# Another hand-written order for the head of a fused attention and gated-MoE kernel, and its last three token tiles grouped one by one

## The chip, the cores and the metric

One core of a Trainium2 chip (trn2). The metric is the time of one execution on the device in microseconds. Three runs of the kernel before took 551.12, 551.37 and 553.83 us; their median, 551.37 us, is the time before. All data are float32; the big products are made of float32r parts.

## What is computed

The reference, cut to what matters:

```python
# q, k, v: (4, 8, 576, 64)
out_d = softmax(scale * mean4(q) @ mean4(k).T) @ mean4(v)        # sequence pooled by 4
out_local = softmax(where(|i - j| < 4, scale * q @ k.T, -1e9)) @ v
x = tokens(repeat4(out_d) + out_local)                           # (2304, 512)
x = (sigmoid(x @ w_gate) * (x @ w_val)) @ w_out                  # d_ff = 1536
logits = x @ phi                                                 # 8 experts x 4 slots
slot_in = softmax(logits, axis=tokens).T @ x
slot_out[e] = relu(slot_in[e] @ w1[e]) @ w2[e]                   # w1, w2: 8 x 512 x 1024
out = softmax(logits, axis=slots) @ slot_out                     # (2304, 512)
```

## The kernel before, in words

**Attention.** The 4 x 8 heads are handled as 16 pairs of heads. A pair is a chain of steps: `Q0 Q1 K0 K1` transpose q and k to head-major form (TensorE, L937; copied out by ScalarE), `pool_Q pool_K pool_V` add up groups of four on GpSimd (L639 to L651), `S0 S1` are the local scores (L944), `Sd` the pooled ones (L952), `mx0 mx1 mxd` the mask and the maxima on VectorE, `ex exd` the exponents on ScalarE, `norm norm_d` the sums and quotients on VectorE, `PT PdT` transposes of the probabilities (L962 to L979), and `PVd PV0 PV1` the products with v (L973, L989), whose sum VectorE writes into `xraw`, a ring of 1152 tokens.

**Feed-forward.** Tokens come in 18 tiles of 128. `xs:i` splits a tile of x into a high and a low part (`xhl`). `gate:i.c` and `val:i.c` are 12 matmuls of 512 columns each (L1036), for one of three 512-wide chunks c of the 1536 columns: x-high by w-high, x-high by w-low, x-low by w-high. ScalarE takes the tanh of gate (L730), VectorE multiplies with val into `hid` (L851). `TR:i.c` transposes hid back (L1046) into `hT`. The weights w_gate and w_val come in 12 pieces of 512 KB (`w_in`), of which `w_hi` (ScalarE, L658) and `w_lo` (VectorE, L839) make the two parts.

**Routing.** w_out is never applied to the tokens. In the head, w_out's 12 pieces (`wo_in`) are transposed (`WT`, L995) and multiplied by phi (`GP`, L1002), and `GS` (L1010) brings that into `gmat`, so that `LG` (L1060) gives a group's logits from `hT` directly. For a group of one or two tiles `LS` (L1070) spreads the logits, VectorE takes a running maximum (L859 to L863), ScalarE the exponents and the factor `alpha` (L752 to L658), `ELT` (L1076) transposes the exponents back, and `SL` (L1085) adds up weighted `hid` per slot, which VectorE adds to `acc` (L879). `LG0` is a part of a group's logits done ahead. The groups before: seven pairs of tiles, then tile 14, tile 15, and tiles 16 and 17 together.

**Experts.** 32 tiles of 1 MB of w1 and w2 stream into 24 places (`ew_low`, `ew_high`), 21 at first and 11 again into places already used. The places lie over the memory of the earlier phases: `wait_place` (L573) lets SP issue a tile once that memory is dead, `first_places` gives the sequence of places. In numbers of places, 7 to 18 are the split weights of gate and val, chunk by chunk, 19 and 20 are `xhl`, and 21 to 23 hT, hid and small tiles. After the last group come the transposes of `acc` (L1110), the product with w_out (L1117), then for each expert `up` (L1136), a transpose (L1146) and the second product (L1154), and in the end 18 output tiles (L1178).

**What sets the order.** Every engine walks one list of steps and takes its part of each. The list begins with the texts `HEAD` (pairs 0 to 4, all of w_out, most weight pieces) and `FIRST_TILE` (token tile 0), both written out step by step. `program_steps` (L72) makes the rest: an alternation of gate and val with the attention of the later pairs between, `put` places the routing steps by hand, and the last three tiles have an order of their own. Loads of the head are steps too: SP issues them in list order, and each waits on SP for what it overwrites (`q_in` for `Q1`, `k_in` for `K1`, `v_in` for `PV1` of the pair before, `v4_in` for `pool_V`, `wo_in` for `WT` four pieces back). `place` (L177) deals PSUM banks to the steps in list order, seven in the head, four after it. `keep_clock` (L901) issues dummy matmuls on TensorE.

```python
put(place_of[("val", (i, c))] + 1, ("TR", (i, c)))
...
def load_wo_piece(sp, f):
    if f >= WO_STAGES:
        wait_unit(sp, ("WT", f - WO_STAGES))
...
for s in head + body[:k]:
    load_step(sp, s)
```

## Time and profile before

| | us |
|---|---|
| median of three runs (551.12, 551.37, 553.83) | 551.37 |
| the profiled execution, its own time | 553.79 |
| its span, from first to last instruction | 552.0 |
| TensorE busy | 528.6 |
| VectorE busy | 225.4 |
| ScalarE busy | 195.8 |
| GpSimd busy | 106.8 |
| mean granted TensorE clock, share of full speed | 0.985 |

The span has three stretches: the head with the first token tile (to 83 us), the feed-forward with attention between (to 484 us), and the routing's end, the experts and the output (to 552 us). An engine's busy time counts all its instructions, with pipelined matmuls counted once. A long wait of an engine that is not the one the end hangs on costs nothing. The profiled execution is longer by 1.8 us than its span, and every duration read from it belongs to its own 553.79 us.

### The profile page before, as it was taken

Reading aid. Unit: us, or ns where it says so; the run is one execution under the profiler, and the core shown is the slowest. Engines: PE = TensorE matmul, PEld = TensorE weight load, DVE = VectorE, ACT = ScalarE, POOL = GpSimd, SP = SyncE. Lnnn points to the kernel's source line nnn. Section 1 sums busy time; section 2 is a strip of 40 time slices with the busy share of each in tenths; the row PEclk is TensorE's granted clock in tenths of the full one; section 3 lists DMA queues with packets and bytes.
Section 4 is the critical chain, followed back from the end, with each engine's and each line's share of the span. In section 5 each row is a group of like instructions: output and inputs, shape, how many; then the busy total and the mean of one; then the engine's idle time right before and its main releaser. Section 6 shows DMA issues by size and latency. Waiting matters only on the chain.

```text
span 552.0 us, 11786 instructions
## 1 busy us (share of the span) xinstructions
PE 528.6 (96%) x4770; PEld 404.1 (73%) x4770; DVE 225.4 (41%) x484; ACT 195.8 (35%) x530; POOL 106.8 (19%) x171
## 2 busy tenths in 40 slices
PE   5989999999999999999999999999999999999982
PEld 4768778877887787878777877878777788854431
DVE  0977965343643446253353527432223110140113
ACT  3757754242443243424233425233122212231022
POOL 8556253221212123112121212100000000000000
PEclk9979999999999999999999999999999999999997
DMA  9966963210311122011111110107006077599959
GB/s 207 231 159 153 341 131 89 67 44 14 77 47 45 45 45 67 23 47 44 47 44 45 45 47 0 27 1 287 18 0 213 17 262 275 215 397 394 400 192 342
DMA packets 86709, 71.00 MB, mean 129 GB/s; under 512 B 61312, under 2 KB 65920, under 8 KB 86656
## 3 DMA queue, kind: packets, MB, share of 16 engines
q1 hardware_dynamic: 86656, 70.25, 41.5%
q8 instruction: 38, 0.62, 0.5%
q14 instruction: 15, 0.12, 0.1%
HBM read 65.52 MB, written 4.72 MB: 127 GB/s over the span
## 4 chain that ended last, share of the span: by engine, by line
PE 85%; DMA 6%; SPq 2%; DVE 2%; issue 1%; ACT 1%; POOL 1%; DVEq 0%; ACTq 0%; POOLq 0%
PE gateb L1036 26%; PE valb L1036 26%; PE unitb L1046 4%; DMA ew_low<-in_moe_w_dram 3%; PE unitb L944 3%; PE unitb L989 3%; PE unitb L937 3%; PE unitb L1060 2%; PE unitb L1085 2%; DMA v<-in_v_dram 2%; PE unitb L973 2%; PE unitb L952 1%; PE unitb L1136 1%; PE unitb L979 1%; PE gateb L1154 1%
## 5 line engine op out<-in xcount | busy, mean ns | idle before, releaser
L1036 PE MATMUL valb<-w_hl,xhl 128*128 128x512 f32 x648 | 162.1, 399 | 0.0
L1036 PE MATMUL gateb<-w_hl,xhl 128*128 128x512 f32 x648 | 161.7, 398 | 0.0
L1036 PEld LDWEIGHTS gateb<-w_hl,xhl 128*128 128x128 f32 x648 | 118.3, 188 | 28.9 <-issue 4.1
L1036 PEld LDWEIGHTS valb<-w_hl,xhl 128*128 128x128 f32 x648 | 118.4, 188 | 25.0 <-issue 1.4
L851 DVE SCALAR_TENSOR_TENSOR hid<-hid,valb 128x512 f32<-128x512 f32 x54 | 37.1, 687 | 121.8 <-PE valb L1036 121.7
L730 ACT ACTIVATE hid<-gateb 128x512 f32<-128x512 f32 x54 | 32.2, 597 | 143.6 <-PE gateb L1036 143.6
L647 POOL TENSOR_TENSOR vd<-v 72x256 f32<-72x256 f32 x16 | 13.6, 850 | 103.6 <-PE unitb L973 87.5
L843 DVE TENSOR_TENSOR xhl<-xraw,xhl 128x512 fp32r<-128x512 f32 x18 | 12.8, 709 | 48.9 <-ACT xhl L658 48.8
L1046 PE MATMUL unitb<-ident,hid 128*128 128x128 f32 x216 | 31.9, 272 | 0.0
L658 ACT ACTIVATE hT<-unitb 128x512 f32<-128x512 f32 x54 | 31.7, 592 | 0.3 <-PE unitb L1046 0.3
L1046 PEld LDWEIGHTS unitb<-ident,hid 128*128 128x128 f32 x216 | 26.5, 140 | 6.8 <-issue 0.4
L639 POOL TENSOR_TENSOR qd<-qT 128x144 f32<-128x144 f32 x16 | 9.5, 596 | 98.1 <-ACT qT L658 97.9
L682 ACT ACTIVATE probd<-unitb,negd 128x144 f32<-128x144 f32 x33 | 12.2, 377 | 34.2 <-DVE negd L793 34.2
L642 POOL TENSOR_TENSOR qd<-qd,qT 128x144 f32<-128x144 f32 x32 | 22.7, 710 | 2.5
L780 DVE TENSOR_TENSOR prob<-unitb,mask 128x350 f32<-128x350 f32 (+1 forms) x24 | 11.5, 481 | 25.0 <-PE unitb L944 24.7
L658 ACT ACTIVATE probT<-unitb 70x64 f32<-70x64 f32 (+1 forms) x45 | 15.1, 338 | 16.4 <-PE unitb L979 16.4
L642 POOL TENSOR_TENSOR kd<-kd,kT 128x144 f32<-128x144 f32 x32 | 19.4, 607 | 2.5
L989 PE MATMUL unitb<-probT,vloc 70*64 70x64 f32 x528 | 18.3, 222 | 0.0
L989 PEld LDWEIGHTS unitb<-probT,vloc 70*64 70x64 f32 x528 | 17.6, 138 | 0.5 <-issue 0.4
L834 DVE TENSOR_TENSOR xraw<-unitb,outd 128x384 f32<-128x384 f32 (+1 forms) x29 | 12.2, 455 | 12.8 <-PE unitb L989 12.8
L944 PEld LDWEIGHTS unitb<-kT,qT 64*64 64x64 f32 x432 | 15.0, 138 | 3.3 <-issue 3.2
L944 PE MATMUL unitb<-kT,qT 64*64 64x70 f32 x432 | 16.9, 229 | 0.0
(179 smaller groups left out, 659.3 us busy)
## 6 DMA issues: line engine op xcount, KB each, us to landing
ew_low<-in_moe_w_dram SPq DMA_DIRECT2D x19, 1024.0 KB, 12.1
ew_high<-in_moe_w_dram SPq DMA_DIRECT2D x13, 1024.0 KB, 8.2
qtok<-in_q_dram SPq DMA_DIRECT2D x32, 144.0 KB, 2.7
ktok<-in_k_dram SPq DMA_DIRECT2D x32, 144.0 KB, 2.9
v<-in_v_dram SPq DMA_DIRECT2D x32, 144.0 KB
out_dram<-outs SPq DMA_DIRECT2D x18, 256.0 KB, 3.0
vloc<-in_v_dram SPq DMA_DIRECT2D x32, 112.0 KB
xraw<-in_moe_w_out_dram SPq DMA_DIRECT2D x12, 256.0 KB, 4.7
```

What stands on the lines that cost most here:

```text
L642: nc.gpsimd.tensor_tensor(dst, dst, src[j], ALU.add).then_inc(step if j == 2 else done, 1)
L647: nc.gpsimd.tensor_tensor(vd[:, :, :, :], v4[:, :, :, 0, :], v4[:, :, :, 1, :], ALU.add).then_inc(vd_step, 1)
L658: return nc.scalar.activation(dst, src, ACT.Copy, scale=scale)
L682: last = nc.scalar.activation(probd[:, t, :], ub[:, t * SD:(t + 1) * SD], ACT.Exp, bias=negd[:, t:t + 1], accum_out=smd[:, t:t + 1])
L730: nc.scalar.activation(hid[:, i % NH, c * CW:(c + 1) * CW], gateb[n % 2][:, :], ACT.Tanh, scale=0.5)\
L843: nc.vector.tensor_tensor(xhl[:, arg % NX, 1, :, :], xraw[:, :, tok:tok + P], xhl[:, arg % NX, 0, :, :].bitcast(F32), ALU.subtract).then_i ...
L851: nc.vector.scalar_tensor_tensor(out=here, in0=here, scalar=1.0, in1=valb[n % 2][:, :], op0=ALU.add, op1=ALU.mult).then_inc(hid_done, 1)
L937: last = nc.tensor.transpose(ub[:, (t - t0) * TT:(t - t0 + 1) * TT], tok[:, t, :, :].rearrange("p h d -> p (h d)"), ident[0:TT, 0:TT])
L944: last = mm(ub[rows, (t - t0) * KW:(t - t0 + 1) * KW], qT[rows, t * QT:(t + 1) * QT], kT[rows, key_start(t):key_start(t) + KW], start=True ...
L989: last = mm(ub[rows, (t - t0) * QT:(t - t0 + 1) * QT], vloc[:, t, h, :], probT[:, t, h * QT:(h + 1) * QT], start=True, stop=True)
L1036: last = mm(bank[:, :], xhl[:, i % NX, x, kk, :], w_hl[:, c, m, w, kk, :], start=j == 0, stop=j == len(order) - 1)
L1046: last = nc.tensor.transpose(ub[:, j * P:(j + 1) * P], hid[:, i % NH, f * P:(f + 1) * P], ident[:])
```

## The change

1. `HEAD` and `FIRST_TILE` are other orders of the same steps. `S0:0` stands behind `WT:0`, the first piece of w_out, where it stood behind `WT:2`; `PT` and `PdT` are mostly written whole; nine weight pieces are loaded ahead of the first gate instead of eleven, and six split instead of eight.
2. The last three tiles (15, 16, 17) are groups of their own, which makes 11 groups. For chunks 1 and 2 of these tiles all gates come first and all vals after them. `first_places` follows: chunk 2's gate weights are freed before chunk 1's val weights.
3. The exponents (`LX`) are a step apart from `LS`, `alpha` has two columns, and `LX` waits for the slot sums of two groups back, not of the last. Some steps of TensorE stand inside the last val step (`inside_items`), after its 4th and 9th matmul. Logits of tile 15 and tile 17 have an `LG0` part; a semaphore `lg_begun` guards the half of `hT` that tile 17 overwrites. Eight dummy matmuls behind `LS` go, four stand behind each of the last two `SL`.

The diff, cut to its core (the second column of `alpha` is used in the same way on VectorE, and TensorE's walk leaves out the steps that stand inside):

```diff
-HEAD = """wo_in:0 wo_in:1 phi_in:0 v4_in:0 Q0:0 wo_in:2 Q1:0 q_in:1 K0:0 WT:0 K1:0 GP:0 WT:1 pool_Q:0 pool_K:0 WT:2 S0:0 Sd:0
-S1:0 mx0:0 mxd:0 k_in:1 exd:0 Q0:1 wo_in:3 Q1:1 GP:1 pool_V:0 K0:1 K1:1 pool_Q:1 mx1:0 wo_in:4 WT:3 norm_d:0 GP:2
-v_in:0 S0:1 wo_in:5 pool_K:1 ex:0 GP:3 WT:4 mx0:1 S1:1 norm:0 WT:5 GS:0 PdT:0 mx1:1 q_in:2 PT0:0 k_in:2 PT1:0 w_in:0
-Sd:1 wo_in:6 ex:1 v4_in:1 mxd:1 K0:2 K1:2 exd:1 w_in:1 Q0:2 PVd:0 norm:1 pool_K:2 Q1:2 w_hi:0 PV0:0 GP:4 S0:2
-norm_d:1 S1:2 mx0:2 wo_in:7 PV1:0 q_in:3 w_hi:1 GP:5 PdT:1 WT:6 WT:7 PT0:1 pool_V:1 mx1:2 k_in:3 ex:2 v_in:1 w_lo:0
-PT1:1 pool_Q:2 Sd:2 v4_in:2 Q0:3 mxd:2 exd:2 K0:3 norm:2 PVd:1 norm_d:2 Q1:3 w_in:2 K1:3 PV0:1 PV1:1 S0:3 GP:6
-w_hi:2 GP:7 S1:3 wo_in:8 mx0:3 w_lo:1 mx1:3 WT:8 PdT:2 pool_K:3 PT:2 pool_Q:3 pool_V:2 ex:3 k_in:4 Sd:3 mxd:3 v_in:2
-exd:3 q_in:4 wo_in:9 GS:1 norm:3 K0:4 wo_in:10 v4_in:3 PVd:2 PV0:2 norm_d:3 wo_in:11 PV1:2 GP:8 K1:4 PT:3 Q0:4 WT:9
-v_in:3 Q1:4 pool_K:4 WT:10 PdT:3 w_in:3 k_in:5 S0:4 mx0:4 GP:9 GP:10 S1:4 w_in:4 pool_V:3 WT:11 PVd:3 w_lo:2 mx1:4
-PV0:3 w_hi:3 GP:11 PV1:3 w_lo:3 w_in:5 pool_Q:4 ex:4 Sd:4 w_in:6 xs:0 w_in:7 GS:2 K0:5 w_hi:4 w_in:8 w_in:9 norm:4
-w_in:10 mxd:4 v4_in:4 w_lo:4 w_hi:5 w_lo:5 exd:4 w_hi:6 w_lo:6 w_hi:7 w_hi:8 w_lo:7 pool_V:4 norm_d:4"""
...
-FIRST_TILE = """gate:0.0 w_hi:9 w_lo:8 w_lo:9 K1:5 w_in:11 val:0.0 PT0:4 gate:0.1 PT1:4 w_hi:10 q_in:5 val:0.1 PdT0:4 v_in:4 v4_in:5
-w_hi:11 w_lo:10 PdT1:4 gate:0.2 TR:0.0 TR:0.1 w_lo:11 pool_K:5 PVd:4 xs:1 Q0:5 val:0.2 PV0:4 PV1:4 k_in:6 v_in:5
-Q1:5 pool_V:5 q_in:6 v4_in:6 pool_Q:5"""
+HEAD = """wo_in:0 wo_in:1 phi_in:0 v4_in:0 Q0:0 wo_in:2 Q1:0 K0:0 K1:0 k_in:1 WT:0 q_in:1 S0:0 WT:1 mx0:0 GP:0 S1:0 pool_Q:0
+mx1:0 pool_K:0 WT:2 ex:0 wo_in:3 Sd:0 K0:1 w_in:0 mxd:0 exd:0 GP:1 pool_V:0 K1:1 Q0:1 wo_in:4 Q1:1 norm:0 k_in:2
+WT:3 GP:2 w_hi:0 S0:1 pool_K:1 GP:3 q_in:2 pool_Q:1 norm_d:0 PdT:0 WT:4 v_in:0 mx0:1 PT:0 wo_in:5 Sd:1 mxd:1 exd:1
+wo_in:6 S1:1 mx1:1 K0:2 PVd:0 ex:1 Q0:2 GS:0 v4_in:1 K1:2 norm:1 Q1:2 PV0:0 GP:4 wo_in:7 WT:5 WT:6 q_in:3 S0:2 GP:5
+norm_d:1 S1:2 pool_Q:2 pool_K:2 k_in:3 mx0:2 WT:7 mx1:2 w_in:1 wo_in:8 GP:6 w_lo:0 PV1:0 v_in:1 PdT0:1 pool_V:1
+PdT1:1 Sd:2 mxd:2 ex:2 wo_in:9 Q0:3 exd:2 norm:2 Q1:3 K0:3 pool_Q:3 norm_d:2 PT:1 K1:3 v4_in:2 q_in:4 k_in:4 PVd:1
+GP:7 WT:8 S0:3 pool_K:3 mx0:3 S1:3 w_hi:1 PV0:1 PV1:1 pool_V:2 v_in:2 PdT:2 mx1:3 Sd:3 mxd:3 PT:2 wo_in:10 exd:3
+GS:1 norm_d:3 PVd:2 ex:3 Q0:4 K0:4 norm:3 Q1:4 w_in:2 K1:4 WT:9 wo_in:11 GP:8 pool_K:4 PV0:2 w_lo:1 w_hi:2 WT:10
+v4_in:3 PV1:2 w_in:3 S0:4 mx0:4 PdT:3 GP:9 pool_Q:4 WT:11 v_in:3 k_in:5 w_hi:3 w_lo:2 w_in:4 S1:4 pool_V:3 mx1:4
+PT:3 w_lo:3 GP:10 Sd:4 GP:11 PVd:3 ex:4 w_in:5 mxd:4 PV0:3 PV1:3 xs:0 w_in:6 w_in:7 w_in:8 exd:4 w_hi:4 GS:2 norm:4
+v4_in:4 w_lo:4 K0:5 w_hi:5 w_lo:5"""
...
+FIRST_TILE = """gate:0.0 norm_d:4 K1:5 val:0.0 pool_K:5 w_hi:6 w_in:9 w_hi:7 w_in:10 w_lo:6 w_lo:7 w_hi:8 gate:0.1 w_in:11 PdT:4
+PT:4 w_hi:9 w_lo:8 q_in:5 w_hi:10 w_hi:11 w_lo:9 pool_V:4 w_lo:10 val:0.1 PVd:4 TR:0.0 w_lo:11 v_in:4 gate:0.2
+TR:0.1 v4_in:5 Q0:5 Q1:5 val:0.2 xs:1 PV0:4 q_in:6 PV1:4 k_in:6 v_in:5 pool_Q:5 pool_V:5 v4_in:6"""
...
-    for c in range(1, chunks):
-        ff += [("gate", (t0, c)), ("val", (t0, c)), ("gate", (t0 + 1, c)), ("gate", (t0 + 2, c)), ("val", (t0 + 1, c)),
-               ("val", (t0 + 2, c))]
...
+    ff += [(name, (i, c)) for name in ("gate", "val") for c in range(1, chunks) for i in range(t0, tiles)]
...
-            for at, name in ((2, "LG"), (3, "LS"), (5, "ELT"), (6, "SL")):
-                put(n + at, (name, g))
...
-    last_c, g = chunks - 1, len(groups) - 3
+            for at, *names in ((2, "LG"), (3, "LS", "LX"), (5, "ELT"), (6, "SL")):
+                put(n + at, *[(name, g) for name in names])
...
+    last_c, g = chunks - 1, len(groups) - 4
...
-    for at, *those in ((1, ("LG", g)), (2, ("LS", g)), (3, ("ELT", g), ("TR", (t0, 0)), ("SL", g)), (6, ("TR", (t0 + 2, 0)))):
+    for at, *those in ((1, ("LG", g)), (2, ("LS", g), ("LX", g)), (3, ("ELT", g), ("TR", (t0, 0)), ("SL", g)), (6, ("TR", (t0 + 1, 0)))):
...
-        n = place_of[("gate", (t0, c))]
-        put(n + 2, ("TR", (t0, c)))
-        put(n + 6, ("TR", (t0 + 2, c)))
-    n = place_of[("gate", (t0, last_c))]
-    for at, *those in ((2, ("TR", (t0, last_c))), (3, ("LG", g + 1)), (4, ("LS", g + 1), *[("TR", (t0 + 1, c)) for c in range(chunks)]),
-                       (5, ("ELT", g + 1), ("LG0", g + 2), ("TR", (t0 + 2, last_c)), ("SL", g + 1)),
-                       (6, ("LG", g + 2)), (7, ("LS", g + 2)), (8, ("ELT", g + 2)), (9, ("SL", g + 2))):
-        put(n + at, *those)
+        put(place_of[("val", (t0, c))] + 1, ("TR", (t0, c)))
+        put(place_of[("val", (t0 + 1, c))] + 1, ("TR", (t0 + 1, c)))
+    n = place_of[("val", (t0, last_c))]
+    put(n - 1, ("LG0", g + 1))
+    put(n, *[("TR", (t0 + 2, c)) for c in range(last_c)], ("TR", (t0, last_c)))
+    put(n + 1, ("LG", g + 1), ("TR", (t0 + 1, last_c)), ("LS", g + 1), ("LX", g + 1), ("LG", g + 2))
+    put(n + 2, ("LS", g + 2), ("ELT", g + 1), ("LG0", g + 3), ("TR", (t0 + 2, last_c)), ("SL", g + 1), ("LX", g + 2), ("LG", g + 3),
+        ("ELT", g + 2), ("LS", g + 3), ("SL", g + 2), ("LX", g + 3), ("ELT", g + 3), ("SL", g + 3))
...
+def inside_items(tiles, chunks, groups_n):
...
+    c, g = chunks - 1, groups_n - 3
+    last = ("val", (tiles - 1, c))
+    return {(last, 4): (("TR", (tiles - 2, c)), ("LS", g)), (last, 9): (("LG", g + 1),)}
...
-    GROUPS = [(i, GT) for i in range(0, TILES - 4, GT)] + [(TILES - 4, 1), (TILES - 3, 1), (TILES - 2, GT)]
+    GROUPS = [(i, GT) for i in range(0, TILES - 4, GT)] + [(i, 1) for i in range(TILES - 4, TILES)]
...
+    inside = inside_items(TILES, FC, GROUPS_T)
...
+    def hT_place(i):
...
+        return 1 if i == TILES - 2 else group_of[i][1]
...
-        g, t = group_of[i]
-        return max((n for n in range(g) if GROUPS[n][1] > t), default=None)
+        return max((group_of[n][0] for n in range(i) if group_of[n][0] < group_of[i][0] and hT_place(n) == hT_place(i)),
+                   default=None)
...
-        first_places = [*range(WO_SLOTS, VAL_HIGH), X_PLACE + 1, VAL_LOW, VAL_HIGH, X_PLACE, *range(X_PLACE + 2, SLOTS)]
+        first_places = [*range(WO_SLOTS, W_PLACE + 6), VAL_HIGH - 2, VAL_HIGH - 1, W_PLACE + 6, W_PLACE + 7,
+                        X_PLACE + 1, VAL_LOW, VAL_HIGH, X_PLACE, *range(X_PLACE + 2, SLOTS)]
...
             elif name == "TR":
                 i, c = arg
                 wait_unit(act, s)
-                t = group_of[i][1]
-                if c == 0 and hT_before(i) is not None:
+                t = hT_place(i)
+                if i == TILES - 1 and c < FC - 1:
+                    act.wait_ge(lg_begun, 1)
+                elif c == (FC - 1 if i == TILES - 1 else 0) and hT_before(i) is not None:
                     wait_unit(act, ("LG", hT_before(i)))
                 copy(hT[:, 4 * c:4 * c + 4, t * P:(t + 1) * P], ub[:, :].rearrange("p (f n) -> p f n", f=4)).then_inc(free, 1)
             elif name == "LG":
...
                     wait_unit(act, ("LS", arg - 1))
                 tok = GROUPS[arg][1] * P
                 copy(l4[:, 0:tok], ub[:, 0:tok]).then_inc(free, 1)
-            elif name == "LS":
+            elif name == "LX":
+                ub, free = banks[at["LS", arg][1]], bank_free[at["LS", arg][1]]
                 act.wait_ge(lmax_step, 3 * arg + 3)
                 if arg > 0:
                     wait_unit(act, ("ELT", arg - 1))
                     act.wait_ge(slot_sum, arg)
-                    wait_free(act, ("SL", arg - 1))
+                if arg > 1:
+                    wait_free(act, ("SL", arg - 2))
                 tok = GROUPS[arg][1] * P
-                nc.scalar.activation(alpha[:], max_step[:], ACT.Exp).then_inc(alpha_done, 1)
+                nc.scalar.activation(alpha[:, arg % 2:arg % 2 + 1], max_step[:], ACT.Exp).then_inc(alpha_done, 1)
                 nc.scalar.activation(el[:, 0:tok], ub[:, 0:tok], ACT.Exp, bias=neg_max[:, arg % 2:arg % 2 + 1],
                                      accum_out=part_sum[:]).then_inc(el_done, 1)
...
-                    nc.vector.scalar_tensor_tensor(out=acc[:, :], in0=acc[:, :], scalar=alpha[:], in1=ub[:, 0:SW],
+                    nc.vector.scalar_tensor_tensor(out=acc[:, :], in0=acc[:, :], scalar=alpha[:, arg % 2:arg % 2 + 1], in1=ub[:, 0:SW],
...
                               start=j == 0, stop=j == len(order) - 1)
                     if j == lows - 1:
                         last.then_inc(low_used, 1)
+                    for between in inside.get((s, j + 1), ()):
+                        pe_step(pe, between)
                 last.then_inc((gate_ready, val_ready)[m], 1)
             elif name == "TR":
                 i, c = arg
...
                 first, size = GROUPS[arg]
                 ub = banks[at["LG", arg][1]]
                 for r in range(FC):
-                    if arg == GROUPS_T - 1 and (r < FC - 1) != (name == "LG0"):
+                    if arg in (GROUPS_T - 1, GROUPS_T - 3) and (r < FC - 1) != (name == "LG0"):
                         continue
                     if r == 0:
                         wait_free(pe, reuse=("LG", arg))
                     wait_free(pe, *[("TR", (first + t, r)) for t in range(size)])
                     for g in range(CG):
                         f = CG * r + g
-                        last = mm(ub[g * NS:(g + 1) * NS, 0:size * P], gmat[:, f, :], hT[:, f, 0:size * P],
+                        last = mm(ub[g * NS:(g + 1) * NS, 0:size * P], gmat[:, f, :], hT[:, f, hT_place(first) * P:(hT_place(first) + size) * P],
                                   start=r == 0, stop=r == FC - 1)
+                if name == "LG0" and arg == GROUPS_T - 3:
+                    last.then_inc(lg_begun, 1)
                 if name == "LG":
                     last.then_inc(unit_ready, 1)
                     if arg == GROUPS_T - 1:
...
-                if arg == GROUPS_T - 1:
-                    keep_clock(8)
...
-                if arg == GROUPS_T - 1:
+                if arg >= GROUPS_T - 2:
```

## Rows read from the trace of the kernel before

**Rows 1.** The page: TensorE's busy time, and the chain by engine
```profile
PE 528.6 (96%) x4770; PEld 404.1 (73%) x4770; DVE 225.4 (41%) x484; ACT 195.8 (35%) x530; POOL 106.8 (19%) x171
...
PE 85%; DMA 6%; SPq 2%; DVE 2%; issue 1%; ACT 1%; POOL 1%; DVEq 0%; ACTq 0%; POOLq 0%
```

**Rows 2.** Windows of the head: busy us and counts, PEclk granted, DMA share, GB/s
```profile
32.00:34.00 2.00, 0.26 (x2) 0.29 (x4) 1.18 (x2) 1.50 (x3) 1.56 (x2) 0.91 0.47 104
34.00:36.00 2.00, 2.00 (x16) 1.62 (x14) 0.52 (x1) 0.00 (x0) 0.00 (x0) 0.50 0.77 196
...
42.00:44.00 2.00, 2.00 (x38) 1.45 (x36) 1.52 (x3) 0.96 (x2) 1.84 (x4) 0.53 0.40 87
```

**Rows 3.** TensorE's timeline, head: start us, length us, instruction, idle before
```profile
11.82 1.43 PE L944 MATMUL gateb<-kT,qT 64*64 64x70 f32 x20
...
28.17 0.57 PE L989 MATMUL unitb<-probT,vloc 70*64 70x64 f32 x12
...
33.74 1.71 PE L952 MATMUL valb<-kd,qd 64*64 64x144 f32 x12 [1.85 <-issue]
...
38.84 2.19 PE L989 MATMUL gateb<-probT,vloc 70*64 70x64 f32 x36
...
48.48 1.22 PE L989 MATMUL unitb<-probT,vloc 70*64 70x64 f32 x36
...
58.58 0.95 PE L952 MATMUL valb<-kd,qd 64*64 64x144 f32 x12 [0.83 <-issue]
...
60.68 2.99 PE L1036 MATMUL gateb<-w_hl,xhl 128*128 128x512 f32 x12
...
83.24 3.01 PE L1036 MATMUL gateb<-w_hl,xhl 128*128 128x512 f32 x12
```

**Rows 4.** GpSimd's timeline, 27 to 34 us
```profile
27.64 1.19 POOL L647 TENSOR_TENSOR vd<-v 72x256 f32<-72x256 f32 x1 [0.37 <-DMA v<-in_v_dram]
...
30.41 1.09 POOL L639 TENSOR_TENSOR qd<-qT 128x144 f32<-128x144 f32 x1
31.58 2.06 POOL L642 TENSOR_TENSOR qd<-qd,qT 128x144 f32<-128x144 f32 x2
```

**Rows 5.** Windows of the tail, columns as in rows 2
```profile
472.00:474.00 2.00, 2.00 (x13) 1.67 (x12) 0.00 (x0) 0.75 (x2) 0.00 (x0) 1.00 0.01 4
...
476.00:478.00 2.00, 2.00 (x30) 1.36 (x29) 0.00 (x0) 0.88 (x2) 0.00 (x0) 1.00 0.28 33
```

**Rows 6.** TensorE's timeline, tail
```profile
476.32 0.86 PE L1060 MATMUL unitb<-hT,gmat 128*32 128x128 f32 x24
...
481.43 3.00 PE L1036 MATMUL valb<-w_hl,xhl 128*128 128x512 f32 x12
...
491.60 1.50 PE L1085 MATMUL unitb<-hid,etok 128*32 128x384 f32 x16 [0.18 <-ACT etok L658]
...
531.70 2.22 PE L1154 MATMUL gateb<-ew_low,hTe 128*32 128x512 f32 x16 [0.28 <-DVE hTe L1222]
```

**Rows 7.** Waits: who waited for whom, us in total, times, longest
```profile
PEld gateb L1154 <- DMA ew_low<-in_moe_w_dram: 1.0, 1, 1.0
```

**Rows 8.** SP's timeline of v's transfers, and the page's row of k's
```profile
28.82 1.38 SPq L521 DMA_DIRECT2D vloc<-in_v_dram  x1
...
32.65 0.32 SPq L527 DMA_DIRECT2D vloc<-in_v_dram  x1
...
ktok<-in_k_dram SPq DMA_DIRECT2D x32, 144.0 KB, 2.9
```

**Rows 9.** VectorE's timeline: the split of a weight piece
```profile
31.10 1.48 DVE L839 TENSOR_TENSOR w_hl<-w_raw,w_hl 128x1024 fp32r<-128x1024 f32 x1
```

**Rows 10.** VectorE's timeline: maximum of the last group
```profile
488.73 0.42 DVE L859 TENSOR_REDUCE part_max<-unitb 128x1 f32<-128x256 f32 x1 [1.14 <-PE unitb L1070]
```

**Rows 11.** DMA issues at 57.8 and 62.5 us: KB, us to landing
```profile
w_raw<-in_moe_w_gate_dram SPq DMA_DIRECT2D x1, 512.0 KB, 12.4
...
w_raw<-in_moe_w_val_dram SPq DMA_DIRECT2D x1, 512.0 KB, 13.5
```

8 lines of the change are left out of this document (5 added, 3 removed).

## The prediction

> **What bounds the kernel now.** I read the page first: TensorE is busy 96% of the span and carries 85% of the chain that ended last; DMA has 6% of it [rows 1]. So a change of order can only pay where TensorE waits, where its clock is down, or where something else ends last. The two-microsecond windows show one such place. In 32 to 34 us TensorE is busy 0.26 us, from 34 to 42 the granted clock is 0.50 (its lower level, 1.2 GHz; the row of 34 to 36 stands for the four windows), 0.53 in 42 to 44 [rows 2]. TensorE's timeline names the step: the pooled scores of pair 2 (`Sd:2`) start at 33.74 after 1.85 us of idling, behind some 2.6 us of nothing but transposes. The price of the clock can be read on one form: 36 probability-by-v matmuls take 2.19 us at 38.84 and 1.22 us at 48.48. A second wait of 0.83 us stands before `Sd:4`; the first gate matmul starts at 60.68, the second token tile at 83.24 [rows 3]. GpSimd's timeline says why `Sd:2` was late: `pool_V:1` waited for its data until 27.64, and `pool_Q:2`, queued behind it, had adds of 1.09 and 2.06 us and ended at 33.64 [rows 4].
>
> The tail has two bounds close together. The expert weights stream without a gap from 476.5; in 472 to 474 the DMA share is 0.01, in 476 to 478 0.28 [rows 5]. TensorE runs from the last FF block through the experts nearly without a break [rows 6], and of all that it waited only 1.0 us for the last weights [rows 7].
>
> **The head, part by part.** Both orders hold the same TensorE steps ahead of the first gate; no instruction is added.
> *The wait at `Sd:2`.* In the new order `pool_Q:2` and `pool_K:2` come before `pool_V:1`, so the pooling behind `Sd:2` no longer hangs on v's transfer. The stall of 1.85 us goes. Next late there is `norm:1`, ahead of `PdT:1`; I find it done before TensorE arrives. Bounds 0 to -1.85; I take -1.85, as the data row's 27.64 has nothing left to hold up.
> *The clock.* It fell after transposes and the stall together [rows 2, 3]. The longest pure run of transposes in the new order is `Q:3 K:3 PT:1`, some 2 us with no stall next to it. If the clock stays up, the gain is half of the time at half clock: 4 windows of 2 us x 0.50 and one of 2 us x 0.47, 4.9 us. Bounds 0 to -4.9; I take all, since without the stall the new order has no stretch as poor as that one.
> *The wait at `Sd:4`.* `pool_Q:4` now follows `S0:4` on the list but its inputs are copied earlier. 0 to -0.8; I take -0.8.
> *What is given back.* Each `v_in` is behind the previous pair's `PV1` on SP, and is six transfers: 28.82 to 32.97, 4.2 us of issuing; a load of the q/k kind needs 2.9 us more to land [rows 8]. So a `PV0` wants 7.1 us between it and the `PV1` before. In the old order pair 1 had 10 us between them (`PV1:0` at 28.17, `PV0:1` at 38.84 [rows 3]). In the new one I count, at the durations of the full clock, about 7.2 us for pair 1 (`PdT Sd Q K PT PVd GP WT S0 S1`), 6.9 for pair 2 and 6.3 for pair 3. That is no slack at all. Bounds 0 to 1.5 us for each of three waits; I take 0.8 each, +2.4. They lie beside matmuls, not beside long runs of transposes, so I let the clock stay up.
> *First scores earlier.* `S0:0` moves ahead of two w_out pieces (it started at 11.82), and VectorE could begin 3 us earlier. But `S1:0`, `S1:1` and the next pairs' loads do not move with it; k's load is now issued ahead of q's, and SP waits for `K1:0` before both. I take 0, with -2 and +1 as ends.
> *The first tile.* `w_in:0` is earlier, and the split of the last weight pieces behind the first gate delays nothing: SP doesn't wait for gates. VectorE's splits take 1.2 to 1.5 us each, one at 31.10 as an example [rows 9], and `w_lo:5` ends about 1 us before `gate:0.1` wants it. 0, and this is a rival below.
> Sum of the head: -1.85 - 4.9 - 0.8 + 2.4 = -5.2 us. So the first gate would start near 55.5 to 56 and the second tile near 78. From there to the last tiles the order is unchanged and TensorE-bound, so the whole lead is kept.
>
> The Trainium skill's SBUF — State Buffer ("SBUF: two separate sides") says that a VectorE instruction with two SBUF inputs locks a shared port against a GpSimd instruction that reads SBUF. The 1.09 us add beside a VectorE subtraction, and the 2.06 us pair beside the 1.48 us split, agree with it [rows 4, 9]. By that rule `pool_Q:2`, which now falls beside `norm:1`'s products instead, could lose some 0.8 us again, and the sum would be -4.4.
>
> **The tail, part by part.** *Weights.* The last gate chunk no longer ends with the 10th of the 12 last FF steps but with the 6th, the second chunk of val with the 9th. Each releases two 1 MB places. Everything released before has landed either way; the gapless stream now starts with the 9th step rather than the 10th. One step is 2.7 to 3.0 us (a step of 3.00 us at 481.43 [rows 6]), and some transposes lie between: the stream starts 3.7 us earlier, at about 472.7, in a stretch where DMA idled [rows 5]. Two short gaps come in (for val's low half and its high half, 1.0 and 0.8 us), so the last weights land about 2 us earlier.
> *Work ahead of the last FF end.* The logits of tile 16 (24 matmuls, 0.86 us for the same form at 476.32) now lie inside the last val step: +0.8.
> *Softmax behind it.* The last group is 128 tokens rather than 256. Its slot sums are 8 matmuls rather than 16, 1.50 to about 0.8 us [rows 6]; maximum 0.42 to 0.3, exponent, copies and logits together another 0.5 [rows 10]. That is -1.4. But three groups are now finished behind the last FF end, not two, and ScalarE copies the last transposed tile only after `ELT:8`'s exponent, which is behind VectorE's maximum of group 9: +0.4. So 0.8 - 1.4 + 0.4 = -0.2 on TensorE's chain. Bounds: -1.4 (the extra group is wholly beside other work) to +3 (it runs in series: from its maximum at 488.73 to its slot sums at 491.60, the old last group took 2.9 us [rows 6, 10]).
> *End.* TensorE 0.2 earlier, weights 2.0 earlier: the 1.0 us wait for the last weights [rows 7] goes as well. -1.2 us. The eight removed dummy matmuls of the old last wait are off the chain; their cover is gone from one softmax wait, and if the clock fell there some 4.9 us would be lost as in the head.
>
> **Sum.** -5.2 - 1.2 = -6.4 us. The profiled execution took 553.79 us (552.0 span and 1.8 around it): 547.4. It is 2.4 us above the median of 551.37. Either those 2.4 are a longer stretch at half clock, which the change removes (547.4 stays), or they lie elsewhere (545.0). I take the middle, **546.2 us**.
>
> **Rivals.** The measurement tells about 0.5%, 2.8 us, from no change: 548.6 and 554.1 are the bounds.
> *A, the forecast*, 0.55: 543 to 548.6. For it: one named stall with a named cause.
> *B, half of the head*, 0.18: the v waits take 1.5 us each and the clock dips once for a few us: a gain of about 1.5 to 3.5, 548 to 550.
> *C, the stall moves*, 0.17 (0.01 of it past the upper bound): `v_in:1`, behind `PV1:0` on SP, is late by 1.5 us or more at `PV0:1`, the clock falls there for as long as before, and the head gains nothing; the tail's 1.2 stays: 550.2. For it: no slack by my count. Against it: the step before `PV0:1` is scores, not transposes.
> *D, slower*, 0.09: the weights are late in the first tile. `w_in:5` is issued at about 53; old pieces of the same crowd landed 12.4 and 13.5 us after issue [rows 11]. With 13 us, a 1.1 us copy and a 1.2 us split it is ready at 68 while `gate:0.1` wants it at 62: a 6 us wait and then about 4.9 us of clock: 551.4 - 6.4 + 10.9 = 555.9. It decides from about 9 us of landing time on. Against it: far fewer pieces stand ahead of `w_in:5` than ahead of those.
> *E*, the change not doing what it says: the orders are literal lists; 0.01.
>
> Faster by over 0.5%: A and a third of B, 0.61; within: the rest of B, C and E, 0.29; slower: D and what C may add by a longer stall, 0.10. The range goes from 543.0 (half of the bounds left in the head, the tail's best) to 551.4 (C with a median's scatter): about 1 in 10 lies on each side.
>
> **What would show it.** Right: no window at clock 0.50 between 30 and 50 us; no wait over 0.5 us before `Sd:2`; first gate matmul (line 1036 there) near 56, the second tile's near 78; the 3-tile issue of ew_high gone in favour of pairs, the DMA share over 0.9 from about 473 with two dents near 481 and 485; no wait for ew_low at the end. Wrong: a wait of TensorE at `PV0:1` to `PV0:3` with a v transfer or SP behind it, half clock at another place, a wait before `gate:0.1`, or more than 10 us from the last val matmul to the transposes of acc.

## The result, and the profile after

The changed kernel took **558.88 us** (median of 4, 557.99 to 561.28) against 551.32 us for the kernel before on the same chip: a ratio of 1.0159, 95% interval 1.0125 to 1.0193. It is slower by 7.6 us where I had forecast 546.2. The profiled execution took 559.26 us, its span 557.5.

The page first (rows of the kernel before: [rows 1]):

```profile
PE 529.8 (95%) x4788; PEld 404.7 (73%) x4788; DVE 228.4 (41%) x495; ACT 195.9 (35%) x537; POOL 107.7 (19%) x171
...
PE 88%; DVE 3%; POOL 2%; issue 2%; DMA 1%; ACT 1%; SPq 0%; ACTq 0%; POOLq 0%; DVEq 0%
```

TensorE is as busy as before. DMA's share of the last chain fell from 6% to 1%, and GpSimd's rose from 1% to 2%. To find the time I cut both profiles at the same two steps: the first gate matmul of the second tile, and the last matmul of the kernel (output projection, 541.14 us before, 545.99 after). What is behind it is the stores of the result.

| us | to second tile | from there to last matmul | from there to the end |
|---|---|---|---|
| before | 83.24 | 457.90 | 10.9 |
| after | 85.37 | 460.62 | 11.5 |

The rows add up to 5.5 us (+2.1, +2.7, +0.6), the medians differ by 7.6. The difference is in the profile of before, which is 2.4 us above its median; e2 below shows where such 2.4 us can lie.

**Head.** TensorE's timeline of the changed kernel (lines have moved: L971 is `Sd`, L992 `PVd`, L1055 gate and val), against [rows 3]:

```profile
31.30 0.95 PE L971 MATMUL valb<-kd,qd 64*64 64x144 f32 x12
...
52.29 0.95 PE L971 MATMUL valb<-kd,qd 64*64 64x144 f32 x12 [0.69 <-issue]
...
56.06 1.23 PE L992 MATMUL unitb<-probdT,vd 72*64 72x144 f32 x8 [2.46 <-POOL vd L666]
...
61.45 5.06 PE L1055 MATMUL gateb<-w_hl,xhl 128*128 128x512 f32 x12
...
85.37 3.02 PE L1055 MATMUL gateb<-w_hl,xhl 128*128 128x512 f32 x12
```

`Sd:2` starts at 31.30 with no wait; before, it was 33.74 after 1.85 us. `Sd:4` starts at 52.29, before at 58.58, but these 6.3 us are not all lead: in the new order `GP:11`, `PVd:3`, `PV0:3` and `PV1:3`, some 2.2 us of work at full clock, come behind it. So the new head is some 4.1 us ahead there. Then `PVd:3` waits 2.46 us for GpSimd's pooled v, and the first gate block takes 5.06 us instead of 2.99. The windows tell why that block is slow (columns as in [rows 2]):

```profile
54.00:56.00 2.00, 0.00 (x0) 0.00 (x0) 1.85 (x2) 0.55 (x3) 1.83 (x2) 0.92 1.09 273
56.00:58.00 2.00, 1.94 (x26) 1.98 (x28) 0.00 (x0) 0.68 (x2) 0.00 (x0) 0.50 1.05 387
...
64.00:66.00 2.00, 2.00 (x6) 1.52 (x6) 1.84 (x4) 0.00 (x0) 0.00 (x0) 0.52 1.04 268
```

The granted clock is 0.50 (1.2 GHz) from the end of that wait until 66 us. Why was the pooled v late? GpSimd's timeline, and VectorE's of the same microseconds:

```profile
46.16 1.11 POOL L654 TENSOR_TENSOR kd<-kT 128x144 f32<-128x144 f32 x1 [3.47 <-ACT kT L673]
47.35 2.29 POOL L657 TENSOR_TENSOR kd<-kd,kT 128x144 f32<-128x144 f32 x2
49.60 0.44 POOL L654 TENSOR_TENSOR qd<-qT 128x144 f32<-128x144 f32 x1
50.12 2.07 POOL L657 TENSOR_TENSOR qd<-qd,qT 128x144 f32<-128x144 f32 x2
52.15 1.30 POOL L662 TENSOR_TENSOR vd<-v 72x256 f32<-72x256 f32 x1
53.53 0.72 POOL L664 TENSOR_TENSOR vd<-vd,v 72x256 f32<-72x256 f32 x1
54.33 1.58 POOL L666 TENSOR_TENSOR vd<-vd,v 72x256 f32<-72x256 f32 x1
```

```profile
46.16 0.81 DVE L831 TENSOR_TENSOR prob<-prob,inv 128x630 f32<-128x630 f32 x1
...
47.35 1.22 DVE L858 TENSOR_TENSOR w_hl<-w_raw,w_hl 128x1024 fp32r<-128x1024 f32 x1
...
49.73 1.39 DVE L858 TENSOR_TENSOR w_hl<-w_raw,w_hl 128x1024 fp32r<-128x1024 f32 x1
...
52.00 0.86 DVE L806 TENSOR_TENSOR prob<-prob,mx 128x630 f32<-128x630 f32 x1
...
53.77 1.56 DVE L858 TENSOR_TENSOR w_hl<-w_raw,w_hl 128x1024 fp32r<-128x1024 f32 x1 [0.32 <-ACT w_hl L673]
```

How long are these adds alone? Later in the same profile VectorE is idle from 79.2 to 84.28, and GpSimd has this row:

```profile
82.42 0.44 POOL L654 TENSOR_TENSOR qd<-qT 128x144 f32<-128x144 f32 x1 [10.04 <-ACT qT L673]
```

The same form takes 1.11 us when it begins with VectorE's product at 46.16. The adds of v take 0.72 (53.53) and 1.58 behind the split that began at 53.77. Each long add begins while VectorE is in an instruction that reads two operands from SBUF. Where GpSimd begins first, its add keeps its length and the split is stretched: the add at 49.60 takes 0.44 and the split at 49.73 takes 1.39, the add at 53.53 takes 0.72 and the split at 53.77 takes 1.56, for 1.22. That is the lock told of in the Trainium skill's SBUF — State Buffer ("SBUF: two separate sides"); the rows agree with it. Against 0.44 and 1.21 for a sum of q or k and 0.72 for an add of v, these sums of pairs 4 and 3 lost some 4.1 us.

**Tail.** TensorE's timeline (L1106 slot sums, L1131 transposes of acc, L1157 first expert product, L1175 second), against [rows 6]:

```profile
487.11 0.96 PE L1055 MATMUL valb<-w_hl,xhl 128*128 128x512 f32 x3
...
491.40 0.85 PE L1106 MATMUL unitb<-hid,etok 128*32 128x384 f32 x8 [1.83 <-ACT el L673]
...
494.10 1.51 PE L1106 MATMUL unitb<-hid,etok 128*32 128x384 f32 x8
...
499.17 0.49 PE L1131 MATMUL unitb<-ident,acc 128*128 128x128 f32 x3
...
505.50 1.93 PE L1157 MATMUL unitb<-ew_low,sT 128*32 128x256 f32 x32
...
536.85 1.92 PE L1175 MATMUL gateb<-ew_low,hTe 128*32 128x512 f32 x16 [0.28 <-DVE hTe L1243]
```

```profile
490.00:492.00 2.00, 0.59 (x8) 0.29 (x12) 0.69 (x4) 1.32 (x6) 0.00 (x0) 1.00 1.02 403
...
494.00:496.00 2.00, 2.00 (x11) 0.68 (x11) 1.79 (x10) 1.05 (x5) 0.00 (x0) 0.50 0.99 388
...
498.00:500.00 2.00, 2.00 (x19) 1.74 (x15) 1.45 (x7) 0.31 (x1) 0.00 (x0) 1.00 0.05 17
```

The 2.7 us of the middle column are three terms. From the second tile to the end of the last val block there are 402.7 us (488.07 - 85.37); before, 401.2 (484.43 - 83.24): +1.5. From there to the first expert product 17.4 instead of 15.9: +1.5. From there to the last matmul 40.5 instead of 40.8: -0.3. In the second term stands a wait of 1.83 us before the slot sums of tile 15 (`SL:8`), the first of the last three groups. The releaser shown is ScalarE's exponent of the *next* group: that exponent is what frees the PSUM bank that the list of banks deals to `SL:8`. Behind it the clock is 0.50, and the next slot sums take 1.51 us instead of 0.85. The weights did come earlier: from 498 to 500 us the DMA share is 0.05 (before, 1.06), with every free place filled and the first expert product not begun.

### The profile page after: what moved, and what is told of

Same layout as the page of the kernel before. It is cut to its first block, busy times and chain, and to the rows that moved or that the text cites. A ratio compares the mean times of both kernels' runs of the same rounds, so it can differ in the third digit from the quotient of the medians.

```text
span 557.5 us, 11853 instructions
## 1 busy us (share of the span) xinstructions
PE 529.8 (95%) x4788; PEld 404.7 (73%) x4788; DVE 228.4 (41%) x495; ACT 195.9 (35%) x537; POOL 107.7 (19%) x171
## 4 chain that ended last, share of the span: by engine, by line
PE 88%; DVE 3%; POOL 2%; issue 2%; DMA 1%; ACT 1%; SPq 0%; ACTq 0%; POOLq 0%; DVEq 0%
PE gateb L1055 28%; PE valb L1055 27%; PE unitb L1067 4%; PE unitb L956 3%; PE unitb L1157 3%; PE gateb L1175 3%; PE unitb L1106 3%; PE unitb L963 2%; PE unitb L1081 2%; PE unitb L1008 2%; PE unitb L992 2%; PE unitb L971 1%; PE unitb L998 1%; DVE outs L1222 1%; DVE w_hl L858 1%
## 5 line engine op out<-in xcount | busy, mean ns | idle before, releaser
L1055 PE MATMUL valb<-w_hl,xhl 128*128 128x512 f32 x648 | 162.8, 400 | 0.5 <-DVE w_hl L858 0.5
L1055 PE MATMUL gateb<-w_hl,xhl 128*128 128x512 f32 x648 | 162.8, 402 | 0.0
L1055 PEld LDWEIGHTS gateb<-w_hl,xhl 128*128 128x128 f32 x648 | 120.1, 190 | 29.4 <-issue 4.1
L1055 PEld LDWEIGHTS valb<-w_hl,xhl 128*128 128x128 f32 x648 | 118.2, 188 | 25.8 <-issue 2.3
L654 POOL TENSOR_TENSOR qd<-qT 128x144 f32<-128x144 f32 x16 | 8.2, 511 | 115.4 <-ACT qT L673 115.3
L662 POOL TENSOR_TENSOR vd<-v 72x256 f32<-72x256 f32 x16 | 12.2, 763 | 87.7 <-PE unitb L992 87.7
L697 ACT ACTIVATE probd<-unitb,negd 128x144 f32<-128x144 f32 x33 | 12.2, 377 | 34.2 <-DVE negd L812 34.2
L799 DVE TENSOR_TENSOR prob<-unitb,mask 128x280 f32<-128x280 f32 (+1 forms) x23 | 11.0, 479 | 23.5 <-PE unitb L963 23.2
L853 DVE TENSOR_TENSOR xraw<-unitb,outd 128x192 f32<-128x192 f32 (+1 forms) x29 | 11.9, 447 | 12.7 <-PE unitb L1008 12.6
L858 DVE TENSOR_TENSOR w_hl<-w_raw,w_hl 128x1024 fp32r<-128x1024 f32 x12 | 16.3, 1385 | 0.3 <-ACT w_hl L673 0.3
L1106 PE MATMUL unitb<-hid,etok 128*32 128x384 f32 x144 | 14.6, 512 | 2.0 <-ACT el L673 1.8
```

The lines of the kernel that those rows point to most:

```text
L858: nc.vector.tensor_tensor(lo, raw, hi.bitcast(F32), ALU.subtract).then_inc(w_lo, 1)
L1055: last = mm(bank[:, :], xhl[:, i % NX, x, kk, :], w_hl[:, c, m, w, kk, :], start=j == 0, stop=j == len(order) - 1)
L1106: last = mm(ub[g * NS:(g + 1) * NS, 0:SW], etok[:, t, :], hid[:, (first + t) % NH, g * SW:(g + 1) * SW], start=t == 0, stop=t == size - 1)
```

## The experiments

Two theories run through them. *Lock and bank*: GpSimd slowed by VectorE makes `PVd:3` late, the bank makes `SL:8` late, and each wait takes the clock along. *Transfers*: the head is bound by its loads, and whatever wait is removed comes back at the next one. Ratios are to the kernel before, run beside each; the runs are from several chips, so ratios are compared and not the times. Expectations are as they stood before each run.

**e1_head_only**: the kernel before, with the two new orders alone.

```diff
-HEAD, FIRST_TILE of the kernel before
+HEAD, FIRST_TILE of the changed kernel
```

> The kernel before with the new HEAD and FIRST_TILE alone. Theory H (the loss starts in the head: pool_V:3 is late for PVd:3, TensorE waits 2.5 us and then runs some 10 us at half clock): the second tile starts near 85 us and the time is 2 to 4.5 us above before, 553.5 to 556. Theory T (the whole loss is in the routing tail): equal to before within 1 us, 551 to 552.

554.83 us, ratio 1.0078 (1.0053 to 1.0102). `PVd:3` waits 2.52 us, the second tile is at 84.94.

**e2_tail_only**: the changed kernel with the two old orders.

```diff
-HEAD, FIRST_TILE of the changed kernel
+HEAD, FIRST_TILE of the kernel before
```

> The changed kernel with the old HEAD and FIRST_TILE. The profile after puts 1.5 us of loss between the second tile and the last FF end and 1.5 us between that and the first expert matmul, less 0.3 at the last weights. Theory H: 3 us above before, 554 to 555. Theory T (all is the tail): 7 us above before, 558 to 559.

554.04 us, ratio 1.008 (1.0043 to 1.0116). Head and tail each cost 0.8%, and their sum is the whole 1.6%. This run also shows how the *old* head varies. Its orders are those of the kernel before, yet its profile reads (GpSimd's first add of v at pair 1, `Sd:2`, second tile; then a window):

```profile
27.25 0.73 POOL L662 TENSOR_TENSOR vd<-v 72x256 f32<-72x256 f32 x1
```

```profile
32.09 0.95 PE L971 MATMUL valb<-kd,qd 64*64 64x144 f32 x12 [0.98 <-issue]
...
80.67 3.01 PE L1055 MATMUL gateb<-w_hl,xhl 128*128 128x512 f32 x12
```

```profile
34.00:36.00 2.00, 2.00 (x48) 1.69 (x44) 1.90 (x5) 1.83 (x10) 0.00 (x0) 1.00 0.82 268
```

Here v had landed, so GpSimd did not wait; in the profile of before it waited 0.37 us for it, to 27.64, and its first add of v (1.19 for 0.73) and the adds of `pool_Q:2` were then stretched [rows 4]. The stall at `Sd:2` is 0.98 us instead of 1.85, the clock stays at 1.00 past it (it falls for some 7 us from 46 on), and the second tile comes at 80.67 instead of 83.24.

So the old head differs from one execution to the next, and the mean granted clock of every execution is on record to say how often. In the profile of before, the half clock of the head takes 5.1 us worth of clock out of 552 (0.009 of the mean) and the time behind the last matmul, when TensorE does nothing, some 3.2 us (0.006). By this estimate an execution with a mean of 0.993 or more has hardly any half clock in its head. Of the 77 runs of the kernel before that stand beside the twelve experiments, 39 are at 0.993 or more, with a median of 549.3 us; the 27 below 0.990 have 552.1. The 0.985 and 553.79 us of the profile that my forecast rested on belong to the second kind. Of the ten runs of e1, the new head, none is above 0.991.

The new tail of this run has the same wait before `SL:8` as the changed kernel, without a fall of the clock behind it (1.00 in 484 to 498 us):

```profile
486.68 0.85 PE L1106 MATMUL unitb<-hid,etok 128*32 128x384 f32 x8 [1.83 <-ACT el L673]
```

**e3_splits_late**: the changed kernel with two splits of weights moved off GpSimd's sums.

```diff
-v4_in:3 PV1:2 w_in:3 S0:4 mx0:4 PdT:3 GP:9 pool_Q:4 WT:11 v_in:3 k_in:5 w_hi:3 w_lo:2 w_in:4 S1:4 pool_V:3 mx1:4
-PT:3 w_lo:3 GP:10 Sd:4 GP:11 PVd:3 ex:4 w_in:5 mxd:4 PV0:3 PV1:3 xs:0 w_in:6 w_in:7 w_in:8 exd:4 w_hi:4 GS:2 norm:4
+v4_in:3 PV1:2 w_in:3 S0:4 mx0:4 PdT:3 GP:9 pool_Q:4 WT:11 v_in:3 k_in:5 w_hi:3 w_in:4 S1:4 pool_V:3 mx1:4
+PT:3 GP:10 Sd:4 GP:11 PVd:3 ex:4 w_in:5 mxd:4 PV0:3 PV1:3 xs:0 w_lo:2 w_lo:3 w_in:6 w_in:7 w_in:8 exd:4 w_hi:4 GS:2 norm:4
```

> The changed kernel with w_lo:2 and w_lo:3 moved behind xs:0. In the profile after, GpSimd's adds of pool_Q:4 and pool_V:3 take 2.07, 1.30 and 1.58 us beside VectorE's splits and the subtraction, where 1.2, 0.72 and 0.72 is their length alone. Theory P (the splits hold GpSimd up): the last add of pool_V:3 ends 1.5 to 2 us earlier, the wait before PVd:3 shrinks from 2.5 to under 1 us, the clock may stay up; 4 to 7 us faster than the changed kernel, 552 to 555. Rival (v's transfer or the number of GpSimd steps is what is late): the wait stays over 2 us and the time within 1 us of the changed kernel's.

556.93 us, ratio 1.0121 (1.0071 to 1.0171): by the ratios half of the head's loss or less, between the two expectations, and not clear of the noise against the changed kernel's 1.0125 to 1.0193. The traces say more. The pooled v is ready at 54.23 instead of 55.91. TensorE:

```profile
54.38 0.71 PE L992 MATMUL unitb<-probdT,vd 72*64 72x144 f32 x8 [1.46 <-POOL vd L666]
...
59.66 4.14 PE L1055 MATMUL gateb<-w_hl,xhl 128*128 128x512 f32 x12
```

The adds at 50.29 and 51.45 are back to 1.22 and 0.72, and the wait shrinks by 1.0 us as the splits leave: it is VectorE's splits that lengthen GpSimd's sums. `w_lo:1` still lies beside `pool_K:4` (1.11 and 2.29 as before). After 1.46 us of waiting the clock was still lost.

**e5_clock_kept**: the changed kernel with 10 spare matmuls (identity by identity, into the step's own bank, which the step then overwrites; the profile counts each as two) ahead of the wait.

```diff
 elif name == "PVd":
+    if arg == 3:
+        for _ in range(10):
+            mm(ub[:, 0:P], ident[:], ident[:], start=True, stop=True)
     pe.wait_ge(vd_done, arg + 1)
```

> The changed kernel with ten dummy matmuls on TensorE ahead of PVd:3's wait for GpSimd, about 2.4 us of work where it idles. Theory H: the granted clock stays at full speed from 50 to 66 us, the first gate takes 2.9 us, not 5.06, and the time falls by 4 to 5 us, to 554 to 555, though PVd:3 is not earlier. Rival (the half clock is not the price, since splits of weights hold the first tile anyway): under 1.5 us gained.

554.71 us, ratio 1.008 (1.005 to 1.011): 0.8% less than the changed kernel, as much as going back to the whole old head gives (e2). TensorE's timeline and windows:

```profile
55.47 2.50 PE L991 MATMUL unitb<-ident 128*128 128x128 f32 x20
57.90 0.71 PE L995 MATMUL unitb<-probdT,vd 72*64 72x144 f32 x8
```

```profile
56.00:58.00 2.00, 2.00 (x20) 1.88 (x20) 0.42 (x1) 0.00 (x0) 0.48 (x1) 1.00 1.00 359
```

No window of the head is below 1.00. `PVd:3` itself is later than in the changed kernel (57.90 for 56.06), and the second tile is earlier (83.01 for 85.37). More of the loss was the clock than the wait.

**e4_slot_sums_own_bank**: the changed kernel, `SL:8` in a bank that is free (and the waits for banks that go with it).

```diff
+                elif s == ("SL", 8):
+                    i = 5
```

> The changed kernel with SL:8 dealt PSUM bank 5 (a gate bank, idle by then) instead of the bank that LS:9 still holds until LX:9. Theory B (the 1.83 us wait behind the last transposed tile is the bank's reuse): SL:8 follows the transposes at once, no idle stretch, the clock stays up, and from the last val matmul to the first expert matmul it takes 15.0 to 16.0 us instead of 17.5; 1.5 to 2.5 us faster than the changed kernel. Rival (ScalarE's exponent is late anyway, and TensorE waits for it one step further on): the wait moves to LG:10 and under 0.5 us is gained.

556.15 us, ratio 1.0105 (1.0075 to 1.0135). TensorE, then a window:

```profile
487.86 0.85 PE L1110 MATMUL gateb<-hid,etok 128*32 128x384 f32 x8
...
501.37 1.93 PE L1161 MATMUL unitb<-ew_low,sT 128*32 128x256 f32 x32
```

```profile
490.00:492.00 2.00, 2.00 (x18) 1.08 (x17) 1.27 (x8) 0.90 (x6) 0.00 (x0) 1.00 1.03 422
```

No wait before `SL:8` (0.40 us are left at the last logits), full clock, and 15.0 us from the end of the last val block (486.42) to the first expert product instead of 17.4. From the second tile to the last matmul it is 458.2 us: 2.4 less than the changed kernel, still 0.3 more than before. e2 divides the 2.4: with the wait and without the fall of the clock it has 459.4, so about 1.2 us are the wait and 1.2 the clock.

**e6_last_logits_first**: the changed kernel, with `SL:8` moved behind the last logits.

```diff
-    put(n + 2, ("LS", g + 2), ("ELT", g + 1), ("LG0", g + 3), ("TR", (t0 + 2, last_c)), ("SL", g + 1), ("LX", g + 2), ("LG", g + 3),
+    put(n + 2, ("LS", g + 2), ("ELT", g + 1), ("LG0", g + 3), ("TR", (t0 + 2, last_c)), ("LX", g + 2), ("LG", g + 3), ("SL", g + 1),
```

> The changed kernel with SL:8 after LG:10 on every engine's list, the banks dealt as before. Theory B: the last logits no longer stand behind the bank's wait, they start 1.4 us earlier, and 1 to 2 us are gained against the changed kernel, though the idle stretch before them remains 1 us or so. Rival (the chain hangs on ScalarE's and VectorE's queues, not on TensorE's order): within 0.5 us.

557.47 us, ratio 1.0114 (1.0063 to 1.0165), not clear of the noise against the changed kernel. The wait changes its place; in front of the last logits it now waits for ScalarE's copy, and 459.2 us lie between the cuts:

```profile
489.53 0.43 PE L1081 MATMUL unitb<-hT,gmat 128*32 128x128 f32 x8 [1.19 <-ACT hT L673]
```

**e7_pool_unlocked_old_tail**: the kernel before with the new orders, all three splits moved (`w_lo:1` ahead of `norm_d:3`, the others as in e3).

```diff
-GS:1 norm_d:3 PVd:2 ex:3 Q0:4 K0:4 norm:3 Q1:4 w_in:2 K1:4 WT:9 wo_in:11 GP:8 pool_K:4 PV0:2 w_lo:1 w_hi:2 WT:10
+GS:1 w_lo:1 norm_d:3 PVd:2 ex:3 Q0:4 K0:4 norm:3 Q1:4 w_in:2 K1:4 WT:9 wo_in:11 GP:8 pool_K:4 PV0:2 w_hi:2 WT:10
```

> The kernel before with the new HEAD and FIRST_TILE, in which w_lo:1 stands ahead of norm_d:3 (where GpSimd idles) and w_lo:2 and w_lo:3 behind xs:0. Theory P: pool_V:3 ends near 53 us, PVd:3 does not wait, no half clock between 50 and 70 us, the second tile starts at 78.5 to 80; 5 to 6 us faster than the new order with the old tail, and level with before or up to 2 us faster. Rival (something else is late by then, such as v's transfer or the first tile's splits): the second tile starts after 82 and the time stays 3 us or more above before.

552.68 us, ratio 1.0038 (1.0013 to 1.0063). Most of GpSimd's adds are back to their short form and `pool_V:3` ends at 53.03; `PVd:3` has no wait. The second tile is at 82.64, not at 78.5 to 80, for TensorE pauses inside `Sd:4`, between its tenth and eleventh matmul:

```profile
53.95 0.40 PE L952 MATMUL valb<-kd,qd 64*64 64x144 f32 x2 [1.53 <-issue]
```

The profile shows nothing that it waits for. The DMA share is 1.11 in 50 to 52 us and 0.84 in 52 to 54. In the changed kernel 0.69 us stand ahead of the same step. The clock falls again, from 57.0 to 63.7. The splits were worth 0.4% (1.0078 in e1), and neither expectation holds in full: `PVd:3` does not wait, but the second tile and the clock are the rival's.

**e8_old_order_q2_first**: the kernel before, with `pool_Q:2` ahead of `pool_V:1` and nothing else.

```diff
-norm_d:1 S1:2 mx0:2 wo_in:7 PV1:0 q_in:3 w_hi:1 GP:5 PdT:1 WT:6 WT:7 PT0:1 pool_V:1 mx1:2 k_in:3 ex:2 v_in:1 w_lo:0
-PT1:1 pool_Q:2 Sd:2 v4_in:2 Q0:3 mxd:2 exd:2 K0:3 norm:2 PVd:1 norm_d:2 Q1:3 w_in:2 K1:3 PV0:1 PV1:1 S0:3 GP:6
+norm_d:1 S1:2 mx0:2 wo_in:7 PV1:0 q_in:3 w_hi:1 GP:5 PdT:1 WT:6 WT:7 PT0:1 pool_Q:2 pool_V:1 mx1:2 k_in:3 ex:2 v_in:1 w_lo:0
+PT1:1 Sd:2 v4_in:2 Q0:3 mxd:2 exd:2 K0:3 norm:2 PVd:1 norm_d:2 Q1:3 w_in:2 K1:3 PV0:1 PV1:1 S0:3 GP:6
```

> The kernel before with pool_Q:2 ahead of pool_V:1 and nothing else. The prediction's cause of the old stall: Sd:2 starts at 32 or before, not at 33.74, the clock stays up from 34 to 44 us, and the kernel is 2 to 5 us faster than before (less where before's own runs lose little clock). Rival (GpSimd's adds are held up by VectorE whichever comes first, or the clock falls anyway behind the transposes): within 1 us of before.

551.41 us, ratio 1.002 (0.9983 to 1.0056): a miss. TensorE's waits:

```profile
31.24 0.95 PE L952 MATMUL valb<-kd,qd 64*64 64x144 f32 x12
...
34.84 1.27 PE L989 MATMUL gateb<-probT,vloc 70*64 70x64 f32 x36 [0.71 <-DMA vloc<-in_v_dram]
...
41.26 0.63 PE L995 MATMUL valb<-ident,xraw 128*128 128x128 f32 x4 [2.46 <-DMA xraw<-in_moe_w_out_dram]
```

The stall is gone and the lead is handed to v's transfer and then to w_out's; the clock falls at the second (0.50 in 44 to 56). Taking away the stall alone is worth nothing by the ratio, and this supports the theory of transfers for the old head. It does no more than that: the profiled execution took 554.83 us, 3.4 above the median, so such waits need not be in every execution.

**e9_unlocked_clock_kept**: e7 with e5's 10 spare matmuls (`w_lo:1` stands ahead of `norm_d:3`, as in e7, not behind it as the expectation says).

```diff
 elif name == "PVd":
+    if arg == 3:
+        for _ in range(10):
+            mm(ub[:, 0:P], ident[:], ident[:], start=True, stop=True)
```

> The new orders with w_lo:1 moved behind norm_d:3 and w_lo:2 and 3 behind xs:0, the old tail, and 10 spare matmuls ahead of PVd:3's wait. Theory A (what is left of the head's loss once GpSimd runs free is the half clock behind its waits): the clock stays at 1.0 from 54 to 64 us, the first gate takes 3.0 us instead of 5.17, the second tile starts near 79.5 instead of 82.64, and the time is 549 to 550.5 (552.7 without the spare matmuls): as the kernel before or up to 0.4% faster. Theory B (transfers and VectorE are late behind it anyway, and the matmuls at half speed only hid that): waits of 1 to 2 us appear at PV0:3, at the first gate or at val 0:0, the second tile starts at 81.5 or later, and the time is 551.5 or more.

555.68 us, ratio 1.0093 (1.0067 to 1.0119): slower than e7 by 3.0 us, a miss. The first gate and val blocks run at full clock, and then:

```profile
59.08 3.01 PE L1039 MATMUL gateb<-w_hl,xhl 128*128 128x512 f32 x12
...
67.00 4.47 PE L1039 MATMUL gateb<-w_hl,xhl 128*128 128x512 f32 x12 [1.94 <-DVE w_hl L839]
```

TensorE now waits at the second gate block until VectorE has split its weights, and loses the clock there. VectorE's rows of these two splits, in e7 and in this run:

```profile
62.89 2.35 DVE L839 TENSOR_TENSOR w_hl<-w_raw,w_hl 128x1024 fp32r<-128x1024 f32 x2
...
63.87 2.98 DVE L839 TENSOR_TENSOR w_hl<-w_raw,w_hl 128x1024 fp32r<-128x1024 f32 x2
```

They end at 65.24 in e7 and at 66.85 here; the block could have begun at 65.06 here and began at 67.02 in e7. So the half clock of e7 had hidden some 0.2 us, and 1.6 us are new. In e7 `PVd:3` had no wait, so that 2.5 us of spare matmuls were in its way: it starts at 56.12, not 54.64, and the first gate block at 59.08 in both. VectorE's chain, which hangs on the products behind `PVd:3`, comes 1.0 us later. And the sum of k of pair 5, now earlier, lies beside the splits: 2.98 us for 2.35.

**e10_old_head_clock_kept**: the kernel before with 10 spare matmuls ahead of the wait of `Sd:2`.

```diff
 elif name == "Sd":
+    if arg == 2:
+        for _ in range(10):
+            mm(ub[:, 0:P], ident[:], ident[:], start=True, stop=True)
     pe.wait_ge(q_pooled, arg + 1)
```

> The kernel before with 10 spare matmuls ahead of Sd:2's wait for the pooled queries. Theory A (the stall at Sd:2 is what takes the clock, and the half clock costs what my prediction said, 4.9 us): full clock from 30 to 44 us, the second tile some 3 to 5 us earlier than 83.24, time 546 to 549. Theory B (the head goes by its transfers, as the run that removed this stall showed; the clock falls at the next wait, for w_out's transfer or v): the clock still falls somewhere between 34 and 46 us or new waits for transfers take its place, the second tile starts between 81.5 and 84.5, time 550 to 552.5.

553.94 us, ratio 1.0046 (1.002 to 1.0073). The clock is kept from 30 to 46 us, and falls then, at `PVd:2`:

```profile
47.13 1.23 PE L976 MATMUL unitb<-probdT,vd 72*64 72x144 f32 x8 [0.58 <-POOL vd L651]
```

```profile
46.00:48.00 2.00, 1.42 (x14) 1.26 (x15) 1.90 (x4) 1.69 (x8) 0.91 (x2) 0.64 0.58 215
```

The second tile is at 84.80. Again nothing is gained. Here too the spare matmuls were in the way: the pooled queries were ready at 34.21, and `Sd:2` starts at 35.40, when the spare matmuls are through.

**e11_both_mended**: the changed kernel with e7's orders, e5's spare matmuls and e4's bank.

```diff
-HEAD, FIRST_TILE of the changed kernel
+HEAD, FIRST_TILE of e7
...
+                elif s == ("SL", 8):
+                    i = 5
...
+    if arg == 3:
+        for _ in range(10):
+            mm(ub[:, 0:P], ident[:], ident[:], start=True, stop=True)
```

> The changed kernel with its three losses mended together: w_lo:1 to 3 moved behind the pooled sums, 10 spare matmuls ahead of PVd:3's wait, and the slot sums of tile 13 in a bank of their own. If the losses add (my reading: head's lock and clock 5.5 us, bank 2.4 to 2.7 us out of 558.9), the time is 550 to 551.5, the second tile starts near 79.5 to 80.5, and 15 us lie between the end of the last val and the first expert matmul. If the new tail costs something in the first-half tiles or the logits beyond these (theory B), it stays at 552 to 554, over the same head with the old tail by 1.5 us or more.

554.52 us, ratio 1.0073 (1.0047 to 1.0099): faster than the changed kernel, but 3 us over my figure. The tail does as expected (458.1 us between the cuts), the head has e9's wait at the second gate block (1.96 us). (`SL:8` is tile 15's, not tile 13's as the expectation has it.)

**e12_weights_first**: e9 with VectorE's `norm:4`, `norm_d:4` and GpSimd's `pool_K:5` moved behind the splits.

```diff
-PT:3 GP:10 Sd:4 GP:11 PVd:3 ex:4 w_in:5 mxd:4 PV0:3 PV1:3 xs:0 w_lo:2 w_lo:3 w_in:6 w_in:7 w_in:8 exd:4 w_hi:4 GS:2 norm:4
-v4_in:4 w_lo:4 K0:5 w_hi:5 w_lo:5"""
-
-FIRST_TILE = """gate:0.0 norm_d:4 K1:5 val:0.0 pool_K:5 w_hi:6 w_in:9 w_hi:7 w_in:10 w_lo:6 w_lo:7 w_hi:8 gate:0.1 w_in:11 PdT:4
+PT:3 GP:10 Sd:4 GP:11 PVd:3 ex:4 w_in:5 mxd:4 PV0:3 PV1:3 xs:0 w_lo:2 w_lo:3 w_in:6 w_in:7 w_in:8 exd:4 w_hi:4 GS:2
+v4_in:4 w_lo:4 K0:5 w_hi:5 w_lo:5 norm:4"""
+
+FIRST_TILE = """gate:0.0 K1:5 val:0.0 w_hi:6 w_in:9 w_hi:7 w_in:10 w_lo:6 norm_d:4 w_lo:7 pool_K:5 w_hi:8 gate:0.1 w_in:11 PdT:4
```

> The run before it with spare matmuls (555.7, second tile 84.15) had its next wait at gate 0:1, 1.94 us for VectorE's w_lo:4 and 5, queued behind norm:4 and stretched by GpSimd's key sums. Here norm:4 stands behind w_lo:5, norm_d:4 behind w_lo:6 and pool_K:5 behind w_lo:7. Theory A (the order of VectorE's queue makes that wait): at most 0.5 us of it is left, the clock stays at 1.0 in 66 to 72 us, the second tile starts at 80.5 to 81.5 and the time is 551 to 553. Theory B (the transfers of the weights are what is late there, whatever VectorE's order): the wait stays over 1.2 us, the clock falls again, the second tile at 83 or later, time 554 or more.

556.26 us, ratio 1.0105 (1.0063 to 1.0147). The second gate block has no wait, so VectorE's order did make it. But:

```profile
68.43 0.45 PE L962 MATMUL unitb<-ident,probd 48*72 48x48 f32 x12 [1.27 <-DVE probd L801]
...
70.10 2.98 PE L1039 MATMUL valb<-w_hl,xhl 128*128 128x512 f32 x12 [0.72 <-DVE w_hl L839]
...
74.69 0.71 PE L976 MATMUL unitb<-probdT,vd 72*64 72x144 f32 x8 [1.60 <-POOL vd L651]
```

```profile
70.62 3.92 POOL L651 TENSOR_TENSOR vd<-vd,v 72x256 f32<-72x256 f32 x1
```

What was moved is late next. A single add of 0.72 us takes 3.92 beside three splits in a row.

## Why the prediction was wrong, point by point

All runs in the cuts of the first table; "tail" is the middle column:

| us | second tile | tail | stores | median | ratio |
|---|---|---|---|---|---|
| e1 new head | 84.94 | 457.67 | 10.9 | 554.83 | 1.0078 |
| e2 new tail | 80.67 | 459.41 | 12.5 | 554.04 | 1.0080 |
| e3 | 82.68 | 460.80 | 11.8 | 556.93 | 1.0121 |
| e4 | 83.78 | 458.20 | 11.7 | 556.15 | 1.0105 |
| e5 | 83.01 | 460.57 | 10.8 | 554.71 | 1.0080 |
| e6 | 84.18 | 459.22 | 12.2 | 557.47 | 1.0114 |
| e7 | 82.64 | 457.95 | 10.9 | 552.68 | 1.0038 |
| e8 | 84.44 | 457.73 | 10.8 | 551.41 | 1.0020 |
| e9 | 84.15 | 457.71 | 12.4 | 555.68 | 1.0093 |
| e10 | 84.80 | 457.78 | 11.7 | 553.94 | 1.0046 |
| e11 | 84.22 | 458.09 | 10.9 | 554.52 | 1.0073 |
| e12 | 85.16 | 457.86 | 11.4 | 556.26 | 1.0105 |

The old tail is 457.7 to 458.0 us in every kernel that has it. The stores vary by 1.7 us with no order in it, and the head of one profile need not be that of the median, so small differences are read from the ratios, each of which is good to 0.25 to 0.5%.

*The wait at `Sd:2`, -1.85, and at `Sd:4`, -0.8.* The first was right as to the place: gone in the changed kernel. Wrong as a gain: e8 removes it alone and wins nothing, and e2 shows that it was 0.98 us in another execution. The second is still there, 0.69 us for 0.83.

*"If the clock stays up, the gain is half of the time at half clock", 4.9.* **This step failed first.** I took the fall of the clock for a consequence of this one stall, with nothing to follow. In the changed kernel the 4.9 us at the old place are gone, and the clock costs 4.7 us behind `PVd:3` and 1.2 in the tail. It falls at one of the later waits: at `PVd:3` (changed kernel, e1, e3, e4, e6), behind the pause in `Sd:4` (e7), at w_out's transfer (e8), at `PVd:2` (e2, e10), at the second gate block (e9, e11), at `PVd:4` (e12). I had also read its price from one execution, 2.4 us above the median. Of the two readings that I gave for those 2.4 us, "a longer stretch at half clock" was the right one (e2 and the clocks of the 77 runs), and by it the whole change could gain 4.0 us at most against the median, not the 5.2 that I took. In about half of the executions of the kernel before there was next to nothing of these 4.9 us to gain.

*The SBUF lock, "could lose some 0.8 us again".* **The second step that failed, and the largest.** I had the mechanism and its rows, and applied it to `pool_Q:2` alone. "VectorE's splits take 1.2 to 1.5 us each" was counted for VectorE, as 0, and never laid beside GpSimd's queue. The new order puts `w_lo:1`, `2` and `3` beside `pool_K:4`, `pool_Q:4` and `pool_V:3`, which stand one behind another: 4.1 us on GpSimd, 2.46 of them a wait of TensorE, and some 9.9 us at half clock behind it, worth 4.7 by the lengths of the steps in it. The runs take these apart: two splits moved give back 0.4% (e3, within the noise), all three 0.4% (e7 against e1), the clock alone 0.8% (e5).

*What is given back at v's transfers, +2.4.* Wrong in place: in the changed kernel no `PV0` waits for v noticeably (0.25 us at 38.52, put down to issue): 0.25 at most of the 2.4. e5 has 0.40 us at `PV0:2` and e7 0.29 at `PV0:3`. The count of slack was right in saying that little is left; v's transfer can be late in the old order as well (0.71 us at `PV0:1` in e8).

*The first tile, 0, and the rivals.* The end was D's (slower, 555.9), the place and mechanism were not: no late landing at `gate:0.1`, so D's nearness is luck. The splits of the first tile are a real bound all the same: `val:0.1` waited 0.55 us in the changed kernel, and e9 1.94 us at `gate:0.1`. VectorE's work ahead of them, not the landing, decides that. In kind, C came nearest: the stall moves and the clock falls there. But it had the wrong step and the wrong cause (`PV0:1` and v, for `PVd:3` and GpSimd) and too small a price.

*Tail: ahead of the last FF end, +0.8.* Measured +1.5. I had the logits of tile 16 (0.86 us) and left out what else is put inside the last val steps. By the rows, an estimate, some 0.8 us are those logits, some 0.3 the last val block itself, which takes 3.15 us in three pieces for 2.8 whole, and the rest lies in several small steps. No run tried it.

*Softmax behind it, -1.4 + 0.4.* **The third step that failed.** Measured +1.5, and -1.0 in e4: so the sum of the work was right (-1.0; its parts, too, where a row shows them: slot sums 0.85, maximum 0.28, a wait of 0.40 for ScalarE's copy), and what I lacked was the bank. Splitting the last group makes one more slot-sum result; I looked for who waits for data, not for which bank the step is dealt and who still reads it. That is a wait of 1.83 us, worth 1.2, and 1.2 us of clock. I had named the clock there as a danger, at 4.9 us, and left it out of the sum.

*The weights' wait, -1.0.* The wait is gone as said, and gave 0.3: of a 1.0 us wait of the weight loads, TensorE's matmuls had felt only 0.3 (2.22 us for the last product before [rows 6], 1.92 now). Even mended, the new tail is worth nothing here: 458.1 to 458.2 us against 457.8.

Open: what TensorE waits for inside `Sd:4` (1.53 us in e7, 0.56 and 1.00 in others); why the clock falls behind a wait in one execution and not in another; what `S0:0`, which started 4.4 us earlier (7.46), was worth; and how far transfers alone would let the head come down. None of the twelve kernels beats the one before; e8 is level with it.

## What to carry to other kernels

When a step is moved, lay it beside what the *other* engines run at that time, not only beside its own queue: here a two-operand VectorE instruction next to a GpSimd chain cost the chain up to nearly its own length (1.08 us for a split of 1.22). When a group is split, walk the list of result banks as well as that of the data. And a stall ahead of a fall of the clock is worth its price only if the step behind it is not late as well: try the removal alone (here one word in a list) before counting the clock as a gain. Where each execution's mean clock is on record, look at how many have the fall at all before pricing it from one profile.

## What was not expected of the hardware

The granted clock fell to 0.50 behind a wait of 1.46 us (e3) and, in e10, behind pauses of 1.00 us before 44.22 and 0.58 before 47.13. Behind the same wait of 1.83 us, at the same step of the same tail, it fell in the changed kernel, in e3 and in e5, and did not in e2; it did not behind 0.98 us in e2's head either. So a wait's length alone did not tell. Spare matmuls held the clock in the two places where they were put. At a real wait they gained 0.8% (e5); where the step had little or nothing to wait for they delayed it and what hangs on it, and the clock fell at a later wait (e9, e10). And the lock can cost far more than one overlap: in e12 one add of 0.72 us took 3.92, from 70.62 to 74.54, beside three splits in a row (70.48 to 73.96), as if GpSimd's instruction had not got between them.
